# Windowed attention and a two-layer ReLU6 block: the matmuls in 64-row halves, two tiles at a time, and the sums copied out by VectorE alone

## The chip, the cores and the metric

The kernel runs on one core of a Trainium2 chip. The metric is the device time of the whole launch, in microseconds (us), as the median of several runs; a profiled execution of the same program shows what each engine did. TensorE (PE; its weight loads are shown as PEld), VectorE (DVE), ScalarE (ACT), GpSimd (POOL) and the queue of SyncE (SP) run side by side and wait for each other by semaphores only.

## What is computed

```python
def _attn_ref(x, weight_gen):            # x (4, 4096, 192), weight_gen (4, 4096, 8, 7)
    w = softmax(weight_gen, axis=-1)     # 7 taps for each token and head
    x_unf = windows of 7 tokens ending at each token, zero before the start
    return np.einsum('bshk,bskhg->bshg', w, x_unf).reshape(4, 4096, 192)

def _moe_ref(x, w_in, w_out):            # x (16384, 192), w_in (192, 2048), w_out (2048, 192)
    h = x @ w_in
    g = h * np.clip(h + 3.0, 0.0, 6.0) / 6.0
    return g @ w_out
```

The output is `_moe_ref` of the attention's result, in float32.

## The kernel before

**Tiling.** 16 pairs of groups (`PAIRS`) are worked through. A pair has 8 tokens on each of 128 partitions, and each of its two halves has 4 of them, 512 token columns (`N`). For a half, the attention's result is transposed to channels x tokens: block a (channels 0 to 127) in `xt_a`, block b (channels 128 to 191) in `xt_b`. The hidden size 2048 is cut into 16 tiles of 128 (`TILES`).

**Split numbers.** TensorE multiplies in float32r, a shortened float32. To keep precision every operand is stored as a high part and a low part (the remainder): `w_in`, `w_out`, `xt_a`, `xt_b`, `g_hi` and `g_lo`. ScalarE writes the high parts by a copy, VectorE the low parts by a subtraction.

**A tile.** `fill` (L464) makes h of a tile in one of four PSUM banks `work` by five matmuls of 512 columns: high x high, high x low and low x high of block a, then two for block b. In `xt_b` 64 rows hold high parts and 64 rows hold low parts, so that the first of these gives high x (high + low), the second low x (high + low). ScalarE takes relu(h + 3) out of the bank (L254), VectorE multiplies min(relu, 6) by h in the bank (`gate`, L350), ScalarE copies the high part to `g_hi` (L264) and VectorE the low part to `g_lo` (L361). `multiply` then adds the tile to four banks `sums`, one for each token: for each a matmul of 384 columns (L482, g_hi by w_out high and low side by side) and one of 192 (L484, g_lo by w_out high, onto the second 192 columns).

**A half.** 18 slots (`GROUP_SLOTS`): twelve tiles, the two transposes TA and TB for the next half (L444), four tiles. TensorE fills slot m + 3 (`AHEAD`), then multiplies slot m; a bank of `work` is free when its low part is done. When the last tile has been multiplied, ScalarE copies the first 192 columns of each `sums` bank times 1/6 into `out_stage` (L281), VectorE adds the second 192 times 1/6 (L381), and SP stores the result. In the next half, TensorE's first matmul into each `sums` bank waits for `out_staged`.

**Beside it.** GpSimd does the attention of the next pair (`attend`, L147 to L158), for which VectorE and ScalarE compute the softmax weights in steps laid at slots 4, 5, 7 and 8 (`SHIFT_AT`, `EXP_AT`, `SUM_AT`, `SCALE_AT`; L325 to L341). Each engine's order is the order in which its program is written; a loop `Fori` runs over the pairs.

Of the kernel before, what the change touches and what calls it, by code (L numbers as in the profile page):

```python
# [6 lines left out]
F32R = mybir.dt.float32r  # L7
# [3 lines left out]

# [13 lines left out]

# [7 lines left out]

# [35 lines left out]
def is_tile(m):  # L69
    return slot(m)[1] not in (TA, TB)  # L70

# [11 lines left out]
def transposes_done(q, m):  # L83

    return 2 + 4 * q + sum(not is_tile(i) for i in range(m + 1))
# [47 lines left out]

def attend(eng, t, prods, accs, half, t0, t1, step, steps, ready):

# [26 lines left out]

# [57 lines left out]

def gpsimd_program(nc, pool, t, s):
# [11 lines left out]
    with pool.Fori(1, PAIRS) as q:  # L233
        for half in range(2):
# [3 lines left out]
            pool.wait_ge(s.transposed, 4 * q - 2 + 2 * half)  # L238
            attend(nc.gpsimd, t, t.pool_prod, t.pool_acc, half, 0, GT, s.pool_step,
                   ATTN_STEPS * (2 * q + half), s.attn_ready)  # L240

def scalar_program(nc, act, dram, t, s):
# [4 lines left out]
    def relu(q, m, last=False):  # L249

        if skipped(m, last) or not is_tile(m):
            return
        act.wait_ge(s.filled, tiles_done(q, m))
# [3 lines left out]
    def hi_part(q, m, last=False):  # L257

        if skipped(m, last):
            return  # L260
        half, what = slot(m)
        if is_tile(m):
            act.wait_ge(s.gated, tiles_done(q, m))
            nc.scalar.copy(t.g_hi[:, m % BANKS, :], t.work[m % BANKS][:]).then_inc(s.g_hi_ready, 1)  # L264
        else:
            act.wait_ge(s.transposed, transposes_done(q, m))
            x_hi(1 - half, what, t.work[m % BANKS])
# [8 lines left out]
    def evacuate(q, half):  # L276

        act.wait_ge(s.stored[half], 16 * q + 16)
        for n in range(GT):
            act.wait_ge(s.sums_ready, GT * (2 * q + half) + n + 1)  # L280
# [3 lines left out]
    def step(q, m, last=False):  # L284
        relu(q, m + 1, last)
        if m == SLOTS - 1 + EVAC_LAG:
            evacuate(q, 0)
        if m == ROUND - 1 + EVAC_LAG:
            evacuate(q, 1)
        hi_part(q, m, last)  # L290
        if m == EXP_AT and not last:
            softmax_exp(q + 1)
# [13 lines left out]
    for i, what in enumerate((TA, TB)):  # L306
        act.wait_ge(s.transposed, i + 1)
        x_hi(0, what, t.work[BANKS - 2 + i])
    w_out_hi(1)
    relu(0, 0)  # L310
    for m in range(FIRST):
        step(0, m)
    with act.Fori(0, PAIRS - 1) as q:
        for m in range(FIRST, FIRST + ROUND):
            step(q, m)
    for m in range(FIRST, ROUND + EVAC_LAG):
        step(PAIRS - 1, m, last=True)

def vector_program(nc, dve, t, s):
# [22 lines left out]
    def gate(q, m, last=False):  # L344

        if skipped(m, last) or not is_tile(m):
            return
        bank = t.work[m % BANKS]
        dve.wait_ge(s.relu_ready, tiles_done(q, m))
        nc.vector.scalar_tensor_tensor(bank[:], t.relu[:, m % 2, :], 6.0, bank[:],  # L350
                                       ALU.min, ALU.mult).then_inc(s.gated, 1)

    def lo_part(q, m, last=False):

        if skipped(m, last):
            return
        half, what = slot(m)
        bank = t.work[m % BANKS]
        if is_tile(m):
            dve.wait_ge(s.g_hi_ready, tiles_done(q, m))  # L360
            nc.vector.tensor_tensor(t.g_lo[:, m % BANKS, :], bank[:], f32(t.g_hi[:, m % BANKS, :]),  # L361
                                    ALU.subtract).then_inc(s.g_lo_ready, 1)
        else:
            dve.wait_ge(s.xt_hi_ready, inputs_split(q, m))
            x_lo(1 - half, what, bank)
# [10 lines left out]
    def evacuate(q, half):  # L376

        for n in range(GT):
            stage = t.out_stage[:, half, n * D:(n + 1) * D]
            dve.wait_ge(s.main_staged, GT * (2 * q + half) + n + 1)  # L380
# [3 lines left out]
    def step(q, m, last=False):  # L384
        gate(q, m + 1, last)
        if m == SLOTS - 1 + EVAC_LAG:
            evacuate(q, 0)
        if m == ROUND - 1 + EVAC_LAG:
            evacuate(q, 1)
        lo_part(q, m, last)  # L390
        if last:
            return
        if m == SHIFT_AT:
            softmax_shift(q + 1)
        if m == SUM_AT:
            softmax_sum(q + 1)
        if m == SCALE_AT:
# [27 lines left out]
    gate(0, 0)  # L425
    w_out_lo(0)
    for m in range(FIRST):
        step(0, m)
    w_out_lo(1)
    with dve.Fori(0, PAIRS - 1) as q:  # L430
        for m in range(FIRST, FIRST + ROUND):
            step(q, m)
    for m in range(FIRST, ROUND + EVAC_LAG):
        step(PAIRS - 1, m, last=True)
# [3 lines left out]
def tensor_program(nc, pe, t, s):  # L438
    def transpose_set(half, what, bank):


        src = t.attn_a if what == TA else t.attn_b
# [195 lines left out]
```

## Time and profile before

| | |
|---|---|
| median of 3 runs | 1226.28 us (1226.02 to 1226.76) |
| span of the profiled execution | 1224.4 us |
| TensorE busy | 1194.6 us, 98% |
| VectorE busy | 803.7 us, 66% |
| ScalarE busy | 634.2 us, 52% |
| GpSimd busy | 690.8 us, 56% |
| moved by DMA | 42.08 MB, 34 GB/s |

The span runs from the first to the last instruction; the run's time holds 1.9 us more. Matmuls overlap in the records, and their ends are modelled: what a matmul costs is read from when the next one starts, not from its duration. The granted TensorE clock was full over all but the last slice of the span.

### The profile page before, as it was taken

To read this page: it belongs to the slowest core of one execution; us is meant where nothing else is said; L and a number is where in the kernel's file an instruction comes from. 1 tells how busy PE (TensorE), PEld (TensorE's weight loads), DVE (VectorE), ACT (ScalarE), POOL (GpSimd) and SP (SyncE) were. 2 spreads that over 40 slices of the span, in tenths; PEclk is the share of its full clock that TensorE was granted. 3 is DMA by queue.
4 is the path that set the end of the run, shared out by engine and by line. 5 is a ranking of instruction groups with operands and counts; after the bars stand their busy time and mean duration, and the time that the engine had idled before them with its cause. 6 is when DMAs were issued, how large, how long until landed. Compare 5 with 4: busy or idle time off the path is not lost.

```text
span 1224.4 us, 19650 instructions
## 1 busy us (share of the span) xinstructions
PE 1194.6 (98%) x6848; PEld 1083.3 (88%) x6848; DVE 803.7 (66%) x1362; ACT 634.2 (52%) x1269; POOL 690.8 (56%) x455
## 2 busy tenths in 40 slices
PE   1999999999999999999999999999999999999998
PEld 1899999999999999999999999999999999998997
DVE  7866657576665766656666575766657666566665
ACT  3455555455555555545555554555555555455554
POOL 7893854909358192762918549094581927729100
PEclk9999999999999999999999999999999999999999
DMA  6101010010101001010010100101010010100000
GB/s 179 46 22 58 20 45 13 20 58 20 58 0 65 14 20 58 0 65 13 20 58 20 45 13 20 58 20 58 0 56 22 20 58 0 65 13 13 13 14 13
DMA packets 12071, 42.08 MB, mean 34 GB/s; under 512 B 1183, under 2 KB 5279, under 8 KB 10139
## 3 DMA queue, kind: packets, MB, share of 16 engines
q1 hardware_dynamic: 12059, 41.93, 9.8%
q8 instruction: 7, 0.11, 0.0%
q14 instruction: 5, 0.04, 0.0%
HBM read 29.34 MB, written 12.58 MB: 34 GB/s over the span
## 4 chain that ended last, share of the span: by engine, by line
PE 96%; DVE 1%; POOL 1%; issue 0%; DMA 0%; ACT 0%; DVEq 0%; ACTq 0%
PE work L464 48%; PE sums L482 32%; PE sums L484 15%; PE work L444 2%; POOL pool_acc L154 0%; POOL pool_prod L152 0%; DVE w_in L404 0%; DMA w_raw<-weight_gen_dram 0%; DVE work L350 0%; DVE w_out L410 0%; DVE g_lo L361 0%; DVE out_stage L381 0%; POOL pool_acc L147 0%; POOL pool_prod L148 0%; DVE xt_b L373 0%
## 5 line engine op out<-in xcount | busy, mean ns | idle before, releaser
L350 DVE SCALAR_TENSOR_TENSOR work<-relu,work 128x512 f32<-128x512 f32 x512 | 355.2, 694 | 402.9 <-ACT relu L254 402.8
L482 PE MATMUL sums<-w_out,g_hi 128*128 128x384 f32 x2048 | 614.1, 356 | 0.7 <-DVE g_lo L361 0.7
L254 ACT ACTIVATE relu<-work 128x512 f32<-128x512 f32 x512 | 306.4, 598 | 554.0 <-PE work L464 549.3
L484 PE MATMUL sums<-w_out,g_lo 128*128 128x192 f32 x2048 | 513.0, 251 | 0.0
L464 PE MATMUL work<-xt_a,w_in 128*128 128x512 f32 x1536 | 449.3, 400 | 2.0 <-DVE xt_b L373 2.0
L482 PEld LDWEIGHTS sums<-w_out,g_hi 128*128 128x128 f32 x2048 | 384.3, 188 | 23.7 <-DVE g_lo L361 1.3
L484 PEld LDWEIGHTS sums<-w_out,g_lo 128*128 128x128 f32 x2048 | 389.8, 190 | 15.8
L361 DVE TENSOR_TENSOR g_lo<-work,g_hi 128x512 fp32r<-128x512 f32 x512 | 349.7, 683 | 2.1
L464 PE MATMUL work<-xt_b,w_in 128*128 128x512 f32 x1024 | 318.1, 392 | 0.0
L264 ACT CAST g_hi<-work 128x512 fp32r<-128x512 f32 x512 | 299.3, 585 | 11.4 <-DVE work L350 11.3
L147 POOL TENSOR_TENSOR pool_acc<-x_in,w_soft 128x768 f32<-128x768 f32 (+1 forms) x32 | 50.0, 1563 | 442.7 <-DVE w_soft L341 429.7
L154 POOL TENSOR_TENSOR pool_acc<-pool_acc,pool_prod 128x768 f32<-128x768 f32 (+1 forms) x160 | 295.6, 1847 | 0.0
L464 PEld LDWEIGHTS work<-xt_a,w_in 128*128 128x128 f32 x1536 | 255.6, 189 | 29.5 <-issue 2.3
L152 POOL TENSOR_TENSOR pool_prod<-x_in,w_soft 128x768 f32<-128x768 f32 (+1 forms) x160 | 249.2, 1557 | 0.0
L464 PEld LDWEIGHTS work<-xt_b,w_in 128*128 128x128 f32 x1024 | 192.8, 188 | 44.8
L148 POOL TENSOR_TENSOR pool_prod<-x_in,w_soft 128x768 f32<-128x768 f32 (+1 forms) x32 | 49.0, 1531 | 0.0
L444 PE MATMUL work<-ident,attn_a 128*128 128x128 f32 x128 | 19.7, 277 | 23.2 <-POOL attn_b L158 23.2
L158 POOL TENSOR_TENSOR attn_a<-pool_acc,pool_prod 128x512 f32<-128x512 f32 (+1 forms) x32 | 40.8, 1274 | 2.5
L381 DVE SCALAR_TENSOR_TENSOR out_stage<-sums,out_stage 128x192 f32<-128x192 f32 x128 | 36.6, 348 | 1.5 <-ACT out_stage L281 1.5
L444 PEld LDWEIGHTS work<-ident,attn_a 128*128 128x128 f32 x128 | 14.5, 143 | 23.2 <-issue 23.2
L281 ACT ACTIVATE out_stage<-sums 128x192 f32<-128x192 f32 x128 | 32.0, 346 | 1.8 <-PE sums L484 1.8
L373 DVE TENSOR_TENSOR xt_b<-work,xt_b 64x256 fp32r<-64x256 f32 x64 | 27.0, 422 | 2.0
(31 smaller groups left out, 203.7 us busy)
## 6 DMA issues: line engine op xcount, KB each, us to landing
x_in<-x_dram SPq DMA_DIRECT2D x15, 1344.0 KB, 6.0
out_dram<-out_stage SPq DMA_DIRECT2D x32, 384.0 KB, 2.8
w_raw<-weight_gen_dram SPq DMA_DIRECT2D x16, 224.0 KB, 3.0
w_out_raw<-moe_w_out_dram SPq DMA_DIRECT2D x1, 1152.0 KB, 13.5
x_in<-x_dram SPq DMA_DIRECT2D x1, 768.0 KB, 5.1
w_in_raw<-moe_w_in_dram SPq DMA_DIRECT2D x1, 768.0 KB, 8.9
w_in_raw<-moe_w_in_dram SPq DMA_DIRECT2D x2, 384.0 KB, 10.3
w_out_raw<-moe_w_out_dram SPq DMA_DIRECT2D x1, 384.0 KB, 6.6
```

What stands on the lines that cost most here:

```text
L147: eng.tensor_tensor(acc, x_tap(0), w_tap(0), ALU.mult).then_inc(step, 1)
L148: eng.tensor_tensor(prod[1], x_tap(1), w_tap(1), ALU.mult).then_inc(step, 1)
L152: eng.tensor_tensor(prod[k % 3], x_tap(k), w_tap(k), ALU.mult).then_inc(step, 1)
L154: eng.tensor_tensor(acc, acc, prod[(k - 1) % 3], ALU.add).then_inc(step, 1)
L254: nc.scalar.activation(t.relu[:, m % 2, :], t.work[m % BANKS][:], ACT.Relu, bias=3.0).then_inc(s.relu_ready, 1)
L264: nc.scalar.copy(t.g_hi[:, m % BANKS, :], t.work[m % BANKS][:]).then_inc(s.g_hi_ready, 1)
L350: nc.vector.scalar_tensor_tensor(bank[:], t.relu[:, m % 2, :], 6.0, bank[:], ALU.min, ALU.mult).then_inc(s.gated, 1)
L361: nc.vector.tensor_tensor(t.g_lo[:, m % BANKS, :], bank[:], f32(t.g_hi[:, m % BANKS, :]), ALU.subtract).then_inc(s.g_lo_ready, 1)
L444: ins = nc.tensor.transpose(bank[:, i * P:(i + 1) * P], src[:, half, i * P:(i + 1) * P], t.ident[:])
L464: ins = nc.tensor.matmul(bank[:], w, x, start=(i == 0), stop=(i == len(products) - 1))
L482: nc.tensor.matmul(t.sums[n][:, 0:2 * D], t.g_hi[:, m % BANKS, cols], t.w_out[:, j, :], start=(j == 0), stop=False)
L484: ins = nc.tensor.matmul(t.sums[n][:, D:2 * D], t.g_lo[:, m % BANKS, cols], t.w_out[:, j, 0:D], start=False, stop=(j == TILES - 1))
```

## The change

**TensorE.** Every matmul now takes 64 rows of its operands: rows 0 to 63 ("upper") or 64 to 127 ("lower"), `ROWS`. Two tiles make a duo. `fill_first(d)` issues the five products of tile 2d from the upper rows alternately with those of tile 2d + 1 from the lower rows; `fill_second(d)` then does the other half of each. The two halves so always write to different banks. The fifth product covers only those 256 columns whose high parts lie in the half's rows (`hi_b`), so that low x low is no longer computed. `multiply` handles (tile, part) items: for two `sums` banks at a time a matmul of each half with 384 columns, then one of each with 192; in the next part the halves trade banks. The transposes are halved in the same way. New waits stand on TensorE for its own earlier work: `filled_first` before `fill_second`, `turned` before each `multiply` but the one that starts a half, and `transposed_first`. A duo runs: wait for the bank, fill_first, multiply, fill_second, multiply. `g_hi` and `g_lo` have six buffers (`G_SLOTS`) for four.

**ScalarE and VectorE.** They work by duos: relu of both tiles, then both copies; both gates, then both low parts. The relu has scale 1/6 and bias 0.5, and the gate takes the minimum with 1. ScalarE no longer touches `sums`; VectorE takes each bank out by one `tensor_reduce` over both 192-column parts. The softmax steps are laid behind duos 2, 3, 4 and 5.

TensorE in the loop, a tile of before (its fill, the first two matmuls of its sums):

```order
L464 MATMUL work<-xt_a,w_in 128x512 x3
L464 MATMUL work<-xt_b,w_in 128x512 x2
L475 REGISTER_ALU
L482 MATMUL sums<-w_out,g_hi 128x384
L484 MATMUL sums<-w_out,g_lo 128x192
```

The same engine of after, the end of a `fill_first` and the `multiply` behind it (L501 and L537 upper and lower, L502 lower; x2 is one of each half):

```order
L501 MATMUL work<-xt_b,w_in 128x512
L502 MATMUL work<-xt_b,w_in 128x512
L501 MATMUL work<-xt_b,w_in 128x2x128
L502 MATMUL work<-xt_b,w_in 128x2x128
L524 ISA
L537 MATMUL sums<-w_out,g_hi 128x384 x2
L540 MATMUL sums<-w_out,g_lo 128x192 x2
```

One matmul has become two alternating ones, and the last product has 2 x 128 columns for 512. The program of TensorE has 1799 instructions for 909, that of the other engines is no longer than it was.

VectorE where the sums of the first half leave, before:

```order
L350 SCALAR_TENSOR_TENSOR work<-relu,work 128x512
L380 ISA
L381 SCALAR_TENSOR_TENSOR out_stage<-sums,out_stage 128x192
L380 REGISTER_ALU
L381 SCALAR_TENSOR_TENSOR out_stage<-sums,out_stage 128x192
```

and after:

```order
L363 ISA
L366 ISA
L367 TENSOR_REDUCE out_stage<-sums 128x192 x2
L366 REGISTER_ALU
L367 TENSOR_REDUCE out_stage<-sums 128x192 x2
L343 REGISTER_ALU
L344 SCALAR_TENSOR_TENSOR work<-relu,work 128x512
```

The four reductions stand ahead of both gates of the duo, where the adds stood between a gate and a low part.

```diff
+ROWS = [slice(0, DB), slice(DB, P)]
+def parts_after(d, second_fill):
+    h = d % HALF_DUOS
+    before, recent, new = 2 * d - 4, 2 * d - 3, 2 * d - 2
+    if second_fill:
+        return {1: [(recent, 1)], 2: [(before, 1), (recent, 1), (new, 0)],
+                TRANSPOSE_DUO: [(recent, 1)], TRANSPOSE_DUO + 1: [(before, 1), (recent, 0)],
+                TRANSPOSE_DUO + 2: [(new, 0)]}.get(h, [(recent, 1), (new, 0)])
+    return {2: [(before, 0), (recent, 0)], TRANSPOSE_DUO + 1: [(before, 0)],
+            TRANSPOSE_DUO + 2: [(recent - 2, 1)]}.get(h, [(before, 1), (recent, 0)])
 # ScalarE
-                             bias=3.0).then_inc(s.relu_ready, 1)
+                             bias=0.5, scale=1.0 / 6.0).then_inc(s.relu_ready, 1)
-            nc.scalar.mul(t.out_stage[:, half, n * D:(n + 1) * D], t.sums[n][:, 0:D],
-                          1.0 / 6.0).then_inc(s.main_staged, 1)
 # VectorE
-            nc.vector.scalar_tensor_tensor(stage, t.sums[n][:, D:2 * D], 1.0 / 6.0, stage,
-                                           ALU.mult, ALU.add).then_inc(s.out_staged, 1)
+            if n % 2 == 0:
+                dve.wait_ge(s.sums_ready, GT // 2 * (2 * q + half) + n // 2 + 1)
+            nc.vector.tensor_reduce(t.out_stage[:, half, n * D:(n + 1) * D],
+                                    t.sums[n][:, 0:2 * D].rearrange("p (o c) -> p c o", o=2),
+                                    AX.X, ALU.add).then_inc(s.out_staged, 1)
 # TensorE
+    def products(m, r):
+        rows = ROWS[r]
+        hi_b = bank.rearrange("p (i o c) -> p i o c", o=2, c=P)[:, :, r, :]
+        return [(bank[:], t.w_in[rows, 0, 0, cols], t.xt_a[rows, half, 0, :]),
+                (bank[:], t.w_in[rows, 0, 0, cols], t.xt_a[rows, half, 1, :]),
+                (bank[:], t.w_in[rows, 1, 0, cols], t.xt_a[rows, half, 0, :]),
+                (bank[:], t.w_in[rows, 0, 1, cols], t.xt_b[rows, half, :]),
+                (hi_b, t.w_in[rows, 1, 1, cols], block_b(t, half, r, r))]
+    def fill_first(q, d, last=False):
+        for i, (upper, lower) in enumerate(zip(products(2 * d, 0), products(2 * d + 1, 1))):
+            nc.tensor.matmul(*upper, start=(i == 0), stop=False)
+            ins = nc.tensor.matmul(*lower, start=(i == 0), stop=False)
+        ins.then_inc(s.filled_first, 1)
+    def fill_second(q, d, last=False):
+        pe.wait_ge(s.filled_first, duos_filled(q, d))
+        both = list(zip(products(2 * d + 1, 0), products(2 * d, 1)))
+        for i, (upper, lower) in enumerate(both):
+            ins_upper = nc.tensor.matmul(*upper, start=False, stop=(i == len(both) - 1))
+            ins_lower = nc.tensor.matmul(*lower, start=False, stop=(i == len(both) - 1))
+    def multiply(q, tiles, odd_first, turns, first=False, by_sets=False):
+        if turns is not None:
+            pe.wait_ge(s.turned, turns)
+        order = [(m, part, group) for m, part in tiles for group in range(2)]
+        if by_sets:
+            order = sorted(order, key=lambda o: o[2])
+        for i, (m, part, group) in enumerate(order):
+            sets = [(n, ROWS[(n + odd_first) % 2]) for n in (2 * group, 2 * group + 1)]
+            for n, rows in sets:
+                if j == 0 and part == 0 and not first:
+                    pe.wait_ge(s.out_staged, GT * 2 * q + GT * (m // SLOTS - 1) + n + 1)
+                nc.tensor.matmul(t.sums[n][:, 0:2 * D], t.g_hi[rows, m % G_SLOTS, n * P:(n + 1) * P],
+                                 t.w_out[rows, j, :], start=(j == 0 and part == 0), stop=False)
+            for n, rows in sets:
+                ins = nc.tensor.matmul(t.sums[n][:, D:2 * D], t.g_lo[rows, m % G_SLOTS, n * P:(n + 1) * P],
+                                       t.w_out[rows, j, 0:D], start=False, stop=last_part)
+    def duo(q, d, last=False):
+        bank_free(q, 2 * d - 3, last)
+        fill_first(q, d, last)
+        starts = d % HALF_DUOS == FIRST_DUO
+        multiply(q, parts_after(d, 0), 1, None if starts else turns_before(q, d, 0), by_sets=starts)
+        fill_second(q, d, last)
+        multiply(q, parts_after(d, 1), 0, turns_before(q, d, 1))
```

## Rows read from the trace of the kernel before

**Rows 1.** The page: span, then busy us (share of the span) and instructions of each engine.
```profile
span 1224.4 us, 19650 instructions
PE 1194.6 (98%) x6848; PEld 1083.3 (88%) x6848; DVE 803.7 (66%) x1362; ACT 634.2 (52%) x1269; POOL 690.8 (56%) x455
```
**Rows 2.** The page: the chain that ended last, shares of the span by engine and line.
```profile
PE 96%; DVE 1%; POOL 1%; issue 0%; DMA 0%; ACT 0%; DVEq 0%; ACTq 0%
PE work L464 48%; PE sums L482 32%; PE sums L484 15%; PE work L444 2%; POOL pool_acc L154 0%; POOL pool_prod L152 0%; DVE w_in L404 0%; DMA w_raw<-weight_gen_dram 0%; DVE work L350 0%; DVE w_out L410 0%; DVE g_lo L361 0%; DVE out_stage L381 0%; POOL pool_acc L147 0%; POOL pool_prod L148 0%; DVE xt_b L373 0%
```
**Rows 3.** The costliest groups: shapes, count | busy us, mean ns of one | idle before.
```profile
L350 DVE SCALAR_TENSOR_TENSOR work<-relu,work 128x512 f32<-128x512 f32 x512 | 355.2, 694 | 402.9 <-ACT relu L254 402.8
L381 DVE SCALAR_TENSOR_TENSOR out_stage<-sums,out_stage 128x192 f32<-128x192 f32 x128 | 36.6, 348 | 1.5 <-ACT out_stage L281 1.5
```
**Rows 4.** Timeline of one tile on TensorE: start us, us it took, engine, line, operands, count.
```profile
429.32 0.88 PE L464 MATMUL work<-xt_a,w_in 128*128 128x512 f32 x3
430.03 0.62 PE L464 MATMUL work<-xt_b,w_in 128*128 128x512 f32 x2
...
430.49 0.33 PE L482 MATMUL sums<-w_out,g_hi 128*128 128x384 f32 x1
...
430.66 0.25 PE L484 MATMUL sums<-w_out,g_lo 128*128 128x192 f32 x1
430.66 0.19 PEld L482 LDWEIGHTS sums<-w_out,g_hi 128*128 128x128 f32 x1
...
430.75 0.36 PE L482 MATMUL sums<-w_out,g_hi 128*128 128x384 f32 x1
430.77 0.19 PEld L484 LDWEIGHTS sums<-w_out,g_lo 128*128 128x128 f32 x1
430.94 0.25 PE L484 MATMUL sums<-w_out,g_lo 128*128 128x192 f32 x1
...
431.60 0.41 PE L464 MATMUL work<-xt_a,w_in 128*128 128x512 f32 x1
```
**Rows 5.** Timeline at the transposes of block a, and their costliest group's mean.
```profile
426.34 0.45 PEld L444 LDWEIGHTS work<-ident,attn_a 128*128 128x128 f32 x4
426.43 0.60 PE L444 MATMUL work<-ident,attn_a 128*128 128x128 f32 x4
...
L444 PE MATMUL work<-ident,attn_a 128*128 128x128 f32 x128 | 19.7, 277 | 23.2 <-POOL attn_b L158 23.2
L444 PEld LDWEIGHTS work<-ident,attn_a 128*128 128x128 f32 x128 | 14.5, 143 | 23.2 <-issue 23.2
```
**Rows 6.** Timeline of a middle tile on all engines: fill, relu, copy, gate, low part.
```profile
448.34 0.62 PE L464 MATMUL work<-xt_b,w_in 128*128 128x512 f32 x2
...
449.00 0.60 ACT L254 ACTIVATE relu<-work 128x512 f32<-128x512 f32 x1 [1.21 <-PE work L464]
...
449.63 0.70 DVE L350 SCALAR_TENSOR_TENSOR work<-relu,work 128x512 f32<-128x512 f32 x1 [1.00 <-ACT relu L254]
...
450.24 0.68 DVE L361 TENSOR_TENSOR g_lo<-work,g_hi 128x512 fp32r<-128x512 f32 x1
```
**Rows 7.** Who waited for whom: us in total, times, longest.
```profile
ACT relu L254 <- PE work L464: 549.3, 445, 2.8
POOL pool_acc L147 <- DVE w_soft L341: 429.7, 14, 31.2
```
**Rows 8.** Timeline where the sums of a half leave.
```profile
442.63 1.00 ACT L281 ACTIVATE out_stage<-sums 128x192 f32<-128x192 f32 x4
...
443.38 1.14 DVE L381 SCALAR_TENSOR_TENSOR out_stage<-sums,out_stage 128x192 f32<-128x192 f32 x4
```
**Rows 9.** Timeline of the end.
```profile
1220.10 1.16 DVE L381 SCALAR_TENSOR_TENSOR out_stage<-sums,out_stage 128x192 f32<-128x192 f32 x4 [1.46 <-ACT out_stage L281]
1220.25 0.25 PE L484 MATMUL sums<-w_out,g_lo 128*128 128x192 f32 x1
```
**Rows 10.** Timeline of the start: first relu, low part of w_out, a wait of TensorE.
```profile
29.20 0.60 ACT L254 ACTIVATE relu<-work 128x512 f32<-128x512 f32 x1 [1.49 <-PE work L464]
...
34.79 3.33 DVE L410 TENSOR_TENSOR w_out<-w_out_raw,w_out 128x2304 fp32r<-128x2304 f32 x1
...
39.36 0.44 PE L482 MATMUL sums<-w_out,g_hi 128*128 128x384 f32 x1 [0.73 <-DVE g_lo L361]
```

More of the change, by code:

```diff
@@ L305, in scalar_program @@
     w_in_hi(1)
-    for i, what in enumerate((TA, TB)):
-        act.wait_ge(s.transposed, i + 1)
-        x_hi(0, what, t.work[BANKS - 2 + i])
+    act.wait_ge(s.transposed_a, 1)
+    x_hi(0, TA, t.work[BANKS - 2])
+    act.wait_ge(s.transposed_b, 1)
+    x_hi(0, TB, t.work[BANKS - 1])
     w_out_hi(1)
-    relu(0, 0)
-    for m in range(FIRST):
-        step(0, m)
+    for d in range(FIRST_DUO):
+        duo(0, d)
     with act.Fori(0, PAIRS - 1) as q:
[L314 to L317, printed above, removed]
+        for d in range(FIRST_DUO, FIRST_DUO + DUOS):
+            duo(q, d)
+    for d in range(FIRST_DUO, FIRST_DUO + DUOS):
+        duo(PAIRS - 1, d, last=True)
 def vector_program(nc, dve, t, s):
@@ L424, in vector_program @@
     w_in_lo(1)
-    gate(0, 0)
     w_out_lo(0)
-    for m in range(FIRST):
-        step(0, m)
+    duo(0, 0)
     w_out_lo(1)
+    for d in range(1, FIRST_DUO):
+        duo(0, d)
     with dve.Fori(0, PAIRS - 1) as q:
[L431 to L434, printed above, removed]
+        for d in range(FIRST_DUO, FIRST_DUO + DUOS):
+            duo(q, d)
+    for d in range(FIRST_DUO, FIRST_DUO + DUOS):
+        duo(PAIRS - 1, d, last=True)
@@ L438, in tensor_program, with transposes @@
 def tensor_program(nc, pe, t, s):
-    def transpose_set(half, what, bank):
+    def transposes(half, what, bank, r):
         src = t.attn_a if what == TA else t.attn_b
-        for i in range(GT if what == TA else GT // 2):
-            ins = nc.tensor.transpose(bank[:, i * P:(i + 1) * P], src[:, half, i * P:(i + 1) * P], t.ident[:])
-        ins.then_inc(s.transposed, 1)
-    def fill(q, m, last=False):
+        rows = ROWS[r]
+        return [(bank[:, i * P + r * DB:i * P + (r + 1) * DB], src[rows, half, i * P:(i + 1) * P], t.ident[rows, rows])
+                for i in range(GT if what == TA else GT // 2)]
@@ L449, in fill, with bank_free @@
+    def bank_free(q, m, last=False):
         if skipped(m, last):
             return
[L451 to L462 removed]
@@ L463, in fill @@
[L463 to L487 removed]
+        if is_tile(m):
+            pe.wait_ge(s.g_lo_ready, tiles_done(q, m))
+        else:
+            pe.wait_ge(s.xt_lo_ready, inputs_split(q, m))
@@ L493, in tensor_program @@
+    transpose_second(0, t.work[BANKS - 2], t.work[BANKS - 1], 1)
     pe.wait_ge(s.w_in_lo, 1)
     pe.wait_ge(s.xt_lo_ready, 3)
-    for m in range(AHEAD + 1):
-        fill(0, m)
+    fill_first(0, 0)
+    fill_first(0, 1)
+    fill_second(0, 0)
+    fill_second(0, 1)
     pe.wait_ge(s.w_out_lo, 1)
-    multiply(0, 0, first=True)
+    multiply(0, [(0, 0)], 1, None, first=True)
     pe.wait_ge(s.w_in_lo, 2)
-    for m in range(1, EARLY):
-        fill(0, m + AHEAD)
-        multiply(0, m)
+    bank_free(0, 1)
@@ L503, in tensor_program @@
+    fill_first(0, FIRST_DUO)
+    multiply(0, [(1, 0)], 1, 1)
+    fill_second(0, FIRST_DUO)
+    multiply(0, parts_after(FIRST_DUO, 1), 0, 2)
     pe.wait_ge(s.w_out_lo, 2)
     with pe.Fori(0, PAIRS - 1) as q:
-        for m in range(EARLY, ROUND + EARLY):
-            fill(q, m + AHEAD)
-            multiply(q, m)
-    for m in range(EARLY, ROUND):
-        fill(PAIRS - 1, m + AHEAD, last=True)
-        multiply(PAIRS - 1, m, last=True)
+        for d in range(FIRST_DUO + 1, FIRST_DUO + 1 + DUOS):
+            duo(q, d)
@@ L514 @@
+    for d in range(FIRST_DUO + 1, DUOS + 2):
+        duo(PAIRS - 1, d, last=True)
 class Semaphores:
```

204 lines of the change are left out of this document (111 added, 93 removed).

## The prediction

> **What bounds the kernel now.** I read the page's busy line first, then the chain, the costliest groups, the timeline of one tile, the waits. TensorE is busy 98% of the span, VectorE 66%, ScalarE 52% [rows 1], and the chain that ended last is 96% TensorE: 48% in the fills (L464), 47% in the sums (L482, L484) [rows 2]. Busy time of pipelined matmuls is no proof, so the timeline is the better witness. In a middle tile the five fill matmuls take from 429.32 to 430.49 us, 1.17 us, and the eight of the sums from there to 431.60, 1.11 us, each starting on the heels of the last [rows 4]. A tile is 2.28 us; 512 tiles are 1167 us of 1224.4. The other engines wait for TensorE: ScalarE 549 us at the relu [rows 7]. So the end moves with TensorE's time per tile and with whatever makes TensorE wait.
>
> Two tile equations give what a matmul costs. A fill is 5 x 512 columns in 1.17 us, 0.234 each; a pair of the sums is 384 + 192 columns in 0.278. With a per column and b per matmul, 512a + b = 0.234 and 576a + 2b = 0.278, so a = 0.423 ns and b = 17 ns. There is a floor below which b isn't the word: the 128-column transposes start (0.60 - 0.28)/3 = 0.107 us apart and their weight loads (0.45 - 0.14)/3 = 0.103 [rows 5], where 128a would be 0.054. A load of weights takes about 0.107 us and the next one of the same rows waits for the matmul ahead of it; the load at 430.66 is followed by one at 430.77 [rows 4]. Even the pairs of the sums lean on it: 384a + 0.107 is 0.27 of their 0.278.
>
> **Part 1, the array in 64-row halves.** Each 128-row matmul becomes two of 64 rows, one in each half, written alternately and into different banks. If the halves run side by side, each half has the chain of loads and matmuls that the whole array had, and one step of a pair costs what one matmul costs now. The sums keep their columns: 4 x 0.278 = 1.11 us a tile. A fill keeps four steps of 512 columns, but the fifth, the low part of the weights with block b, now covers 256 columns, because each half takes only the high parts: low times low is dropped. Its price by a and b is 256a + 17 ns = 0.126 us; the bounds are 0.107 (the load) and 0.234 (the strided destination eats it all). I take 0.126, as the trace shows no reason for more: saved 0.108 us a tile, 512 x 0.108 = 55 us. Bounds of this term: 0 to 65 us.
>
> What the trace can't show is a 64-row matmul: [rows 4] has only whole-array ones. From below, b disappears under the other half's work; from above, halves don't overlap at all. Both are rivals below.
>
> Transposes: 6 a half before, 12 with 64 columns after. At 0.107 a step they cost the same if the halves overlap (6 steps); if not, 6 x 0.107 x 32 = 21 us more. I take nothing, as for the rest.
>
> New waits on TensorE. A bank must not be written by both halves at once, so each duo of tiles waits for filled_first and twice for turned. What each waits for lies one block back: between fill_first and fill_second stands a multiply of 0.56 to 1.1 us, between two multiplies a fill of 1.06, where a release takes 0.2 us (last fill matmul starts at 448.57, may stream 0.22, relu starts at 449.00 [rows 6]). Price nothing; at the shortest cover, 0.56 us, a release of 0.2 is still hidden. If that cover were gone it would be 0.2 x 3 x 256 duos, 150 us.
>
> **Part 2, duos.** Both tiles of a duo are filled together, at three quarters of the duo's time. The chain behind it: relu; gate 0.63 later; the next gate 0.60 after that; the copy of the second tile after its gate, 0.6; its low part 0.7 [rows 3, 6]. Written out from the fill's last column: 0.2 + 0.63 + 0.60 + 0.73 + 0.61 + 0.70 = 3.5 us for the odd tile, 2.9 for the even one. TensorE next wants the even low part after a multiply half, the next duo's fill, multiply and second fill: a whole duo (4.34 us) plus half a tile; and the odd one, for the bank, 1.1 + 4.34 = 5.4 us on. Cover 1.9 us, so nothing. What may be laid on top: the softmax steps, now one after each of duos 2, 4 and 5, are 1.3, 1.4 and 0.6 us of VectorE; x_lo 1.5. VectorE's own pace is 4 x 0.60 = 2.4 us a duo against 4.34 [rows 6], so each is caught up within a duo. GpSimd gets the softmax weights some three tiles (7 us) later; it waits 31 us a pair of halves for them now [rows 7], and its first half is needed some 20 tiles later against 22 us of work. Nothing.
>
> **Part 3, the sums leave by VectorE alone.** Off the list go four ScalarE copies and four VectorE adds of 192 elements a half; in come four reductions of 384. From 348 ns for 192 elements and 694 for 512 [rows 3] the slope is 1.08 ns, so 0.56 us each, starting 0.48 apart (0.27 now, (1.14 - 0.35)/3 [rows 8], plus 0.21). This is the one place where TensorE now waits. Let t be when the first two banks of sums end. Banks are free at t + 0.2 + 0.56 = 0.76, then 1.24, 1.72, 2.20. TensorE does the other two banks (0.28) and fill_first (1.06), asks for banks 0 and 1 at t + 1.34, and after two tiles' halves on them (0.56) for 2 and 3 at t + 1.90: the last comes at about 2.2, a wait of 0.3. Over 31 changes of half: 9.5 us. Before, the copy and add pipeline of 0.27 left no such wait [rows 8]. VectorE is held 2 us with the gates of the duo just filled queued behind; that duo's low parts come at 5.4 instead of 3.5, just inside the cover. The bounds: 0 if the reductions start 0.37 apart; 58 us if the stride of 192 elements in PSUM doubles them (rival D). The 1/6 moves from the copies to the relu's scale: same instruction, nothing.
>
> **Head and tail.** The first relu came after one fill [rows 10]; now fill_first of two duos and fill_second of one stand before it, three tiles of filling, and the low part of w_out (3.33 us) stands before duo 1's gates. TensorE was waiting 0.73 us there already [rows 10]. I count 2 us. At the end the last reductions come 0.5 us later than the adds [rows 9].
>
> **Sum, forecast A.** 1224.4 - 55 + 9.5 + 2 + 0.5 = 1181.4 us of span. The runs' median lies 1.9 above the span (1226.28), so 1183.
>
> **The rivals.**
> B, the fixed costs hide. While one half changes weights the other streams, so b goes: fill 2304 x 0.423 = 0.975 us; the pairs of the sums can't go below 384a + 0.107 = 0.27, so 1.08; a tile 2.055, 0.225 saved, 115 us. The wait at the change of half grows to 0.45 us (14). Time 1224.4 - 115 + 14 + 2.5 + 1.9 = 1128. For it: b isn't streaming. Against it: each half still has its own chain of load, matmul, load.
>
> C, slower: the loads queue. Twice as many loads of 128 columns, and if the loads of both halves go through one loader at 0.107 us, a pair of the sums has four of them, 0.43 us instead of 0.278; 1.71 a tile. A step of the fill has two, 0.21, under 0.234, so 4 x 0.234 + 0.21 = 1.15. A tile 2.86, 0.58 more, 297 us; transposes 21 more: about 1545. It decides as soon as loads of different halves are closer than 0.278/4 = 0.07 us apart at best. For it: no loads stand closer than 0.10 in [rows 5] and the loader is busy 6848 x 0.107 = 733 us now, 1470 then. Against it: all loads there fill the same 128 rows, each waits for the matmul before it, so they don't show one loader.
> The Trainium skill ("TensorE: Matmul & The Clock Gate", section LDWEIGHTS) has a load take columns / 1.2 ns whatever the number of rows, which the transposes' 0.107 agrees with; by that page alone halving the rows saves nothing on a load. The Trainium skill ("TensorEngine Tiling (Array Packing)", Key Properties) says that different tiles execute LdWeights and Matmul in parallel, which speaks for A; no run shown here has two tiles.
>
> D, the reductions are slow. A stride of 192 in PSUM at double price, 0.88 us apart: the last bank is free at 0.2 + 3 x 0.88 + 0.96 = 3.8, a wait of 1.9, 31 times 59 us instead of 9.5: 1232. It decides from about 0.4 us apart.
>
> E, feeding. Twice the matmuls through one queue. The closest two matmuls of these kinds start 0.08 to 0.09 apart [rows 4]; if that were the least for any two, the sums take 16 x 0.088 = 1.41 us instead of 1.11 and the fill 10 x 0.088 is still under 1.06: 0.3 - 0.108 more a tile, 98 us: 1325. Against it: those 0.09 are explained by columns and load.
> The Trainium skill ("TensorE: Matmul & The Clock Gate", Part 2, decode and dispatch) prices a decoded matmul at about 62 ns in the sequencer; by it 26 take 1.6 us a tile, and that would not bind at 2.17.
>
> F, the halves don't overlap: 26 matmuls one after another, 10 + 16 at today's spacings, 4.3 us a tile: 2250.
>
> **How the numbers follow.** A 0.44, B 0.18, D 0.09, E 0.10, C 0.15, F 0.04. The likeliest is A, 1183; it alone spans 1160 to 1205. The range is to leave out no more than 2 in 10: C and F are out, so from 1105 (B with a little more) to 1335 (E). A measurement of this kernel tells 0.2%, 2.5 us, from no change. Faster: A, B and some of D's milder forms, 0.66; within 0.2%: a corner of D, 0.03; slower 0.31.
>
> **What would show it.** Right: steps of the fill 0.23 apart in pairs that start within a few ns, the last 0.13; pairs of the sums 0.28; one wait of 0.3 us a half at L537 for VectorE. B: fill steps at 0.217. C: loads never under 0.1 apart, sums at 0.43. D: reductions over 0.9 us and waits of 2 us. E: all matmuls 0.088 apart. The forecast is wrong from the root if paired starts don't coincide.

## The result: 1.8% slower, and the profile after

| | before | changed |
|---|---|---|
| median | 1226.18 us (4 runs, 1226.02 to 1226.76) | 1248.03 us (4 runs, 1241.88 to 1255.40) |
| ratio, 95% interval | | 1.018, 1.014 to 1.022 |
| span of the profiled execution | 1224.4 us | 1239.9 us |

The forecast was 1183 us with 0.66 for faster. The time lies inside the range (1105 to 1335) and on the wrong side of no change. The changed kernel also scatters by 13 us where the old one scatters by 0.7.

The page after: its span and busy lines, the queue q8, which brings in instructions, and its chain. The first two lines answer to [rows 1], the last to [rows 2]; q8 had moved 7 packets for the kernel before:

```profile
span 1239.9 us, 33575 instructions
PE 1169.6 (94%) x13696; PEld 1094.8 (88%) x13696; DVE 841.8 (68%) x1362; ACT 633.3 (51%) x1141; POOL 690.7 (56%) x455
...
q8 instruction: 139, 2.28, 0.8%
...
PE 92%; DVE 4%; ACT 2%; issue 1%; POOL 1%; DMA 0%; DVEq 0%
```

TensorE is busy for 25 us less although the span is 15.5 us longer: its work became shorter, and time without work appeared. First the work. Two steps of a fill and the first matmuls of the sums, in the timeline (start us, us, engine, line, operands), which answers to [rows 4]:

```profile
430.80 0.39 PE L501 MATMUL work<-xt_a,w_in 64*128 64x512 f32 x1
...
430.81 0.39 PE L502 MATMUL work<-xt_a,w_in 64*128 64x512 f32 x1
...
431.03 0.39 PE L501 MATMUL work<-xt_a,w_in 64*128 64x512 f32 x1
...
431.49 0.27 PE L501 MATMUL work<-xt_b,w_in 64*128 64x256 f32 x1
...
431.50 0.27 PE L502 MATMUL work<-xt_b,w_in 64*128 64x256 f32 x1
...
431.60 0.34 PE L537 MATMUL sums<-w_out,g_hi 64*128 64x384 f32 x2
431.61 0.19 PEld L540 LDWEIGHTS sums<-w_out,g_lo 64*128 64x128 f32 x2
431.78 0.26 PE L540 MATMUL sums<-w_out,g_lo 64*128 64x192 f32 x2
...
431.87 0.36 PE L537 MATMUL sums<-w_out,g_hi 64*128 64x384 f32 x2
```

The two halves start 0.01 us apart, so they do run side by side. A step of the fill is 0.23 us, the last 0.11; a pair of the sums (384 and 192 columns) is 0.27 here and 0.28 in the mean of the block before it. The sums here start at 431.60 and those of the previous block at 429.43: a tile is 2.17 us, which is the forecast's number (2.28 - 0.108).

Now the time without work. This is the timeline of TensorE where its loop over the pairs turns, from the last matmul of one turn to the first of the next:

```profile
343.95 0.24 PE L540 MATMUL sums<-w_out,g_lo 64*128 64x192 f32 x1
346.68 0.49 PE L501 MATMUL work<-xt_a,w_in 64*128 64x512 f32 x1 [2.48 <-DVE g_lo L349]
346.68 0.50 PE L502 MATMUL work<-xt_a,w_in 64*128 64x512 f32 x1
```

There are 14 such stops, one for each jump back (15 turns, and the last one's branch isn't taken), of 2.3 to 3.3 us from the start of one matmul to the start of the next, 38 us in all. Nothing in [rows 4 to 10] foretold them. The waits name two causes for them (who waits <- for whom: us in all, count, longest):

```profile
PEld work L501 <- DVE g_lo L349: 33.1, 36, 2.9
PE work L501 <- DVE g_lo L349: 26.4, 11, 2.6
...
PEld work L501 <- issue: 11.7, 4, 3.3
PE work L501 <- issue: 8.5, 3, 3.0
```

11 stops are put down to VectorE's low parts, 3 to "issue". Stops that come at the same place in every turn should have one cause; which, was the first question.

### The profile page after: what moved, and what is told of

It reads as the page before. It is cut to its first block, busy times and chain, and to the rows that moved or that the text cites. A ratio compares the mean times of both kernels' runs of the same rounds, so it can differ in the third digit from the quotient of the medians.

```text
span 1239.9 us, 33575 instructions
## 1 busy us (share of the span) xinstructions
PE 1169.6 (94%) x13696; PEld 1094.8 (88%) x13696; DVE 841.8 (68%) x1362; ACT 633.3 (51%) x1141; POOL 690.7 (56%) x455
## 2 busy tenths in 40 slices
DMA packets 12202, 44.24 MB, mean 36 GB/s; under 512 B 1183, under 2 KB 5279, under 8 KB 10139
## 3 DMA queue, kind: packets, MB, share of 16 engines
q8 instruction: 139, 2.28, 0.8%
## 4 chain that ended last, share of the span: by engine, by line
PE 92%; DVE 4%; ACT 2%; issue 1%; POOL 1%; DMA 0%; DVEq 0%
PE sums L537 35%; PE work L501 19%; PE work L515 18%; PE sums L540 11%; PE work L516 5%; PE work L502 3%; DVE g_lo L349 2%; DVE work L344 1%; ACT g_hi L266 1%; ACT relu L261 1%; PE work L453 1%; PE work L466 1%; POOL pool_acc L166 0%; POOL pool_prod L164 0%; DVE w_in L402 0%
## 5 line engine op out<-in xcount | busy, mean ns | idle before, releaser
L537 PE MATMUL sums<-w_out,g_hi 64*128 64x384 f32 x4096 | 664.5, 356 | 4.0 <-DVE g_lo L349 3.3
L540 PE MATMUL sums<-w_out,g_lo 64*128 64x192 f32 x4096 | 577.2, 249 | 0.0
L344 DVE SCALAR_TENSOR_TENSOR work<-relu,work 128x512 f32<-128x512 f32 x512 | 331.0, 692 | 323.0 <-ACT relu L261 320.4
L261 ACT ACTIVATE relu<-work 128x512 f32<-128x512 f32 x512 | 278.3, 596 | 447.7 <-PE work L516 447.7
L537 PEld LDWEIGHTS sums<-w_out,g_hi 64*128 64x128 f32 x4096 | 474.9, 185 | 25.8 <-DVE out_stage L367 6.9
L540 PEld LDWEIGHTS sums<-w_out,g_lo 64*128 64x128 f32 x4096 | 476.7, 187 | 0.0
L501 PE MATMUL work<-xt_a,w_in 64*128 64x512 f32 x768 | 230.8, 407 | 37.3 <-DVE g_lo L349 26.4
L164 POOL TENSOR_TENSOR pool_prod<-x_in,w_soft 128x768 f32<-128x768 f32 (+1 forms) x160 | 248.3, 1552 | 0.0
L502 PE MATMUL work<-xt_a,w_in 64*128 64x512 f32 x768 | 231.3, 407 | 0.0
L516 PE MATMUL work<-xt_a,w_in 64*128 64x512 f32 x768 | 226.5, 401 | 0.0
L515 PE MATMUL work<-xt_a,w_in 64*128 64x512 f32 x768 | 226.1, 400 | 0.0
L501 PEld LDWEIGHTS work<-xt_a,w_in 64*128 64x128 f32 x768 | 123.9, 187 | 53.4 <-DVE g_lo L349 33.1
L502 PE MATMUL work<-xt_b,w_in 64*128 64x512 f32 (+1 forms) x512 | 130.1, 334 | 0.0
L501 PE MATMUL work<-xt_b,w_in 64*128 64x512 f32 (+1 forms) x512 | 130.0, 333 | 0.0
L515 PEld LDWEIGHTS work<-xt_a,w_in 64*128 64x128 f32 x768 | 123.7, 186 | 6.3
L516 PE MATMUL work<-xt_b,w_in 64*128 64x512 f32 (+1 forms) x512 | 129.2, 331 | 0.0
L515 PE MATMUL work<-xt_b,w_in 64*128 64x512 f32 (+1 forms) x512 | 129.1, 331 | 0.0
L502 PEld LDWEIGHTS work<-xt_a,w_in 64*128 64x128 f32 x768 | 123.9, 187 | 0.1
```

Source lines behind the costliest of these rows:

```text
L164: eng.tensor_tensor(prod[k % 3], x_tap(k), w_tap(k), ALU.mult).then_inc(step, 1)
L501: nc.tensor.matmul(*upper, start=(i == 0), stop=False)
L502: ins = nc.tensor.matmul(*lower, start=(i == 0), stop=False)
L515: ins_upper = nc.tensor.matmul(*upper, start=False, stop=(i == len(both) - 1))
L516: ins_lower = nc.tensor.matmul(*lower, start=False, stop=(i == len(both) - 1))
L537: nc.tensor.matmul(t.sums[n][:, 0:2 * D], t.g_hi[rows, m % G_SLOTS, n * P:(n + 1) * P], t.w_out[rows, j, :], start=(j == 0 and part == 0), ...
```

## Two theories

**Theory 1, the fetch.** TensorE's program doubled, from 909 to 1799 rows, and with it the body of its loop. The engine no longer holds all of it; when the loop jumps back, its first block has to be brought in again. q8's 139 packets of 16 KB are the sign.

**Theory 2, VectorE.** The four reductions stand before the gates of the duo ahead of the loop's end, so the low parts come late and TensorE waits for its bank.

Against theory 2 speaks the middle of each pair: the same reductions stand there too, and TensorE doesn't stop. The trace speaks against it too. These are the last low parts before the stop's end (346.68):

```profile
344.54 1.29 DVE L349 TENSOR_TENSOR g_lo<-work,g_hi 128x512 fp32r<-128x512 f32 x2
```

They are done at 345.83, 0.85 us before TensorE goes on. At the 14 stops this lead is 0.4 to 1.4 us, so it isn't the low part that ends them.

## Experiments on the stops

**The loop written out.** The edit, in TensorE's program only:

```diff
-    with pe.Fori(0, PAIRS - 1) as q:
+    for q in range(PAIRS - 1):
         for d in range(FIRST_DUO + 1, FIRST_DUO + 1 + DUOS):
             duo(q, d)
```

> The changed kernel with TensorE's loop over the pairs written out, so that its program never jumps back; nothing else differs. Theory 1 (fetch): the changed trace stops TensorE for 2.3 to 3.3 us once a pair, 15 times, right after the loop's last matmul, and the instruction queue q8 moved 139 packets where it moved 7; the body no longer stays in the instruction memory. Written out, the stops go: 15 x 2.6 = 39 us less, about 1205 us, and faster than the kernel before. Theory 2 (VectorE): the profile puts 26.4 us of these stops down to the low parts g_lo; then writing out changes nothing and the time stays at 1242 to 1255 us with a stop each pair.

Measured: 1200.3 us (4 runs, 1199.15 to 1203.59), ratio to before 0.980 (0.978 to 0.981). The page and its queue:

```profile
span 1197.3 us, 32405 instructions
PE 1162.8 (97%) x13696; PEld 1101.6 (92%) x13696; DVE 841.8 (70%) x1362; ACT 633.8 (53%) x1141; POOL 690.9 (58%) x455
...
q8 instruction: 107, 1.75, 0.6%
```

Theory 2 falls: VectorE does the same work in the same order (841.8 us), and the stops are gone, with 48 us of median. The 107 packets, in a trace without a stop, show that bringing in code costs nothing visible by itself: written out, all of it is fetched, but in a straight line. What costs is the jump.

**Control: the same edit on the kernel before.**

> Control: the kernel before with the same loop of TensorE written out. Its page had 7 packets on q8 and its pairs follow each other every 74.42 us without a stop, so both theories expect no change, 1226 us. If it gets faster, the kernel before paid at its loop's end too; if it gets slower, a written-out program costs something by itself.

Measured: 1226.19 us, ratio 1.000 (0.999 to 1.001). The old loop cost nothing at its end. Written out, it moves 53 packets on q8; the 7 of the looped kernel lie before 111 us and behind 1170 us, none of them between the jumps.

**The kernel before with a long body.** Three pairs in the body, 5 turns:

```diff
-    with pe.Fori(0, PAIRS - 1) as q:
-        for m in range(EARLY, ROUND + EARLY):
-            fill(q, m + AHEAD)
-            multiply(q, m)
+    with pe.Fori(0, (PAIRS - 1) // 3) as q3:
+        for i in range(3):
+            for m in range(EARLY, ROUND + EARLY):
+                fill(3 * q3 + i, m + AHEAD)
+                multiply(3 * q3 + i, m)
```

> The kernel before with three pairs in the body of TensorE's loop and 5 turns for 15: the same instructions in the same order, but a body of about 2800 instructions instead of 940. Theory 1: each of the 5 turns (4 or 5 jumps back) stops TensorE for 2 to 3 us, 10 to 13 us in all, about 1238 us, and q8 moves well over a hundred packets. Theory 2: no change, 1226 us.

Measured: 1230.08 us, ratio 1.003 (1.002 to 1.004): slower by 3.7 us, a third of what was expected. Four stops appear, one at each jump, in a kernel that had none (0.7, 0.8, 0.7 and 1.2 us from start to start), with 66 packets on q8. So the length of the body is enough, but a jump costs 0.9 us here and 3.4 in the changed kernel (47.7 / 14), with stops of 0.9 and 2.7 on the mean. Why, the branch's own row shows. For one source line the profile gives op, count, shortest/median/longest ns and the first and last start. The kernel before, then this one, then the changed kernel:

```profile
L505 PEldq COMPARE_BRANCH  x15: 76/208/247, 114.5 to 1156.2; - x15
```
```profile
L505 PEldq COMPARE_BRANCH  x5: 83/3296/3780, 263.6 to 1160.1; - x5
```
```profile
L575 PEldq COMPARE_BRANCH  x15: 83/3838/4365, 114.8 to 1169.0; - x15
```

The branch takes 0.2 us where its target is at hand, 3.3 to 4.4 us where it isn't, and 0.08 us on the last turn, when it isn't taken. Two more records tie the stop to the branch. At each of the 14 jumps of the changed kernel a packet of q8 starts 0.9 to 1.1 us behind the start of the branch. And the first matmul starts 0.16 to 0.17 us after the branch ends, at one of the 14 0.23 us. While the branch waits, TensorE works off what its queue holds. In this kernel the first branch starts at 263.6 us and TensorE runs dry after the matmul at 266.34:

```profile
266.34 0.25 PE L484 MATMUL sums<-w_out,g_lo 128*128 128x192 f32 x1
267.13 0.95 PE L464 MATMUL work<-xt_a,w_in 128*128 128x512 f32 x3 [0.53 <-issue]
```

That is 2.7 us of queued work; in the changed kernel the branch of the stop above starts at 342.68 and the last matmul at 343.95, 1.3 us. In both, 16 or 17 matmuls start between the start of the branch and the stop. So the halved matmuls hurt twice: the body grew beyond what is held, and the same number of queued instructions covers half as much of the fetch.

**The same in the fastest kernel.** It is the changed kernel with TensorE's loop written out and the old way out of the sums (1188 us, see below), with the loop put back, three pairs in a body:

> The fastest kernel so far (1188 us: written out, old way out of the sums) with TensorE's loop put back, three pairs in its body: 5 turns, 4 jumps back. If the cost is one fetch for each jump taken, it is 4 x 2.6 = 10 us, and up to 4 x 3.7 = 15 us where the stop also halves the clock for a while: 1198 to 1203 us, with four branches of 3 to 4 us and the fifth, not taken, short. If the cost went with the length of the body or with the number of blocks fetched, it would be near that of the body of one pair, 1243 us.

Measured: 1203.85 us, ratio 0.982 (0.980 to 0.984), 15.7 us above the same kernel written out. Its branch:

```profile
L585 PEldq COMPARE_BRANCH  x5: 83/3627/3862, 256.0 to 1128.5; - x5
```

Four jumps cost 3.9 us each, 14 cost 3.4 us each in the changed kernel (47.7 / 14), 3.9 each with the old way out of the sums (1243.2 - 1188.1 = 55 / 14). The cost goes with the jumps taken, not with the code fetched: 119 packets here, 107 written out. The expectation of 1198 to 1203 us was missed by 1 us.

Part of it is the clock. Stretches of the changed kernel's span, with the granted clock as the third column from the end, before, behind and after one stop:

```profile
180.00:191.20 11.20, 11.20 (x132) 10.19 (x128) 8.44 (x16) 5.67 (x11) 0.00 (x0) 1.00 0.38 146
194.95:198.30 3.35, 3.35 (x26) 3.15 (x25) 0.00 (x0) 0.00 (x0) 0.00 (x0) 0.53 0.00 0
200.00:210.00 10.00, 10.00 (x130) 9.37 (x127) 7.70 (x14) 6.06 (x11) 0.00 (x0) 1.00 0.01 2
```

Behind the stop of 191.1 to 193.7 us TensorE stood at 1.2 GHz for 3.4 us, half of 2.4, which costs it up to 1.7 us. Two of the 14 stops of this execution were followed by such a stretch (those of 2.6 us; the longest, 3.3 us, was not). The four runs' times go with their mean granted clock: 1241.9 us at 0.996, 1247.9 and 1248.2 at 0.990, 1255.4 at 0.981. This is where the scatter comes from, and it is why the 48 us of median are more than the 38 us of stops.

## Experiments on the rest of the change

**The old way out of the sums, in the loop.** ScalarE copies 192 columns, VectorE adds 192, the 1/6 stays in the gate:

```diff
+            nc.scalar.copy(t.out_stage[:, half, n * D:(n + 1) * D], t.sums[n][:, 0:D]).then_inc(s.main_staged, 1)
...
-            nc.vector.tensor_reduce(t.out_stage[:, half, n * D:(n + 1) * D],
-                                    t.sums[n][:, 0:2 * D].rearrange("p (o c) -> p c o", o=2),
-                                    AX.X, ALU.add).then_inc(s.out_staged, 1)
+            dve.wait_ge(s.main_staged, GT * (2 * q + half) + n + 1)
+            nc.vector.scalar_tensor_tensor(stage, t.sums[n][:, D:2 * D], 1.0, stage,
+                                           ALU.mult, ALU.add).then_inc(s.out_staged, 1)
```

> The changed kernel with the old way out of the sums: ScalarE copies the first 192 columns, VectorE adds the second 192 (the 1/6 stays in the gate). If the four reductions of VectorE are what makes TensorE wait at the change of half (0.25 us in the trace) and what puts its two row halves 0.09 us out of step for the following duos (0.066 us a duo), some 0.25 to 0.6 us a half come back: 8 to 19 us less than the changed kernel run beside it (about 1242 to 1248), while the stops at the loop's end stay. If the stops at the loop's end were made by the reductions ahead of the gates (theory 2), they shrink too: up to 39 us more.

Measured: 1243.17 us (1240.15 to 1248.46), ratio 1.014 (1.011 to 1.018). That is 5 us under the changed kernel, less than the 8 to 19 expected, and inside its scatter: by itself inconclusive. Its clock says why:

```profile
core 0: 1240.2 us, clock 0.984
```

All its four runs lie between 0.976 and 0.986. In the profiled execution nine of the 14 stops were followed by a stretch at half clock, one of them twice as long, 34 us in all. Here is the first and the long one:

```profile
118.80:122.10 3.30, 3.30 (x26) 3.06 (x24) 0.00 (x0) 0.00 (x0) 0.00 (x0) 0.50 0.00 0
...
569.40:576.10 6.70, 6.13 (x36) 5.42 (x38) 0.32 (x1) 0.00 (x0) 0.00 (x0) 0.50 0.01 2
```

The changed kernel had two such stretches, 6.8 us. The 27 us more at half clock cost up to 14 us, about what the old way out of the sums gives back below (12 us). Why more stops are followed by a slow stretch here stays open; their length doesn't decide it (2.3 to 3.3 us in both kernels). With the stops gone the part can be read:

**The old way out of the sums, written out.**

> The changed kernel, TensorE's program written out, with the old way out of the sums (ScalarE copies, VectorE adds). Theory: the reductions cost a wait of 0.25 us at each change of half and leave the two row halves 0.09 us out of step, 0.066 us a duo until the next transposes; both go, 0.3 to 0.6 us a half, 10 to 19 us: 1181 to 1190 us against about 1200. Rival: the steps out of step come from something else (the order by sets), and nothing changes.

Measured: 1188.13 us (1186.30 to 1189.53), ratio 0.969 (0.967 to 0.970), the fastest kernel of the study. The way out of the sums costs the written-out kernel 12 us. One change of half with the old way, on all engines:

```profile
362.57 0.26 PE L550 MATMUL sums<-w_out,g_lo 64*128 64x192 f32 x2
362.59 0.99 ACT L281 COPY out_stage<-sums 128x192 f32<-128x192 f32 x4 [2.04 <-PE sums L550]
...
362.94 1.15 DVE L378 SCALAR_TENSOR_TENSOR out_stage<-sums,out_stage 128x192 f32<-128x192 f32 x4 [1.67 <-ACT out_stage L281]
```

The four banks are free 1.5 us after the first copy starts, at 364.09 (362.94 + 1.15). Four reductions take 1.95 us, here in the changed kernel's timeline:

```profile
338.61 1.95 DVE L367 TENSOR_REDUCE out_stage<-sums 128x192 f32<-128x384 f32 x4 [1.31 <-PE sums L540]
```

In the written-out kernel that keeps the reductions TensorE waits for a bank at each change of half, by its waits:

```profile
PEld sums L537 <- DVE out_stage L367: 7.3, 31, 0.3
```

That is 7.3 / 31 = 0.24 us each, and it has a sequel. The bank that comes last belongs to one row half, so that only that half waits. Its timeline at one change of half (the reductions start at 327.07), in front of the wait, behind it, and eight microseconds later:

```profile
327.63 0.39 PE L501 MATMUL work<-xt_a,w_in 64*128 64x512 f32 x1
327.63 0.39 PE L502 MATMUL work<-xt_a,w_in 64*128 64x512 f32 x1
...
329.08 0.18 PEld L537 LDWEIGHTS sums<-w_out,g_hi 64*128 64x128 f32 x1 [0.23 <-DVE out_stage L367]
...
329.56 0.42 PE L516 MATMUL work<-xt_a,w_in 64*128 64x512 f32 x1
...
329.73 0.41 PE L515 MATMUL work<-xt_a,w_in 64*128 64x512 f32 x1
...
337.26 0.39 PE L502 MATMUL work<-xt_a,w_in 64*128 64x512 f32 x1
...
337.36 0.39 PE L501 MATMUL work<-xt_a,w_in 64*128 64x512 f32 x1
```

A pair of matmuls, one of each half, starts together before the wait, 0.17 us apart behind it, and still 0.10 apart eight microseconds on. From transposes to transposes a half takes 36.16 us with the reductions and 35.80 with the old way (mean of 30 each): 0.36 a half. 0.24 of it is the wait; the rest I put down to the ends of the blocks, where one half idles for the skew, which no run took apart.

**The reductions alone, in the kernel before.**

> The kernel before with part 3 alone: 1/6 in relu and gate, VectorE takes each bank of sums by one reduction, ScalarE no longer touches them. Theory: in the old order TensorE asks for a bank 1.2 us after its sums end, one bank each 0.28 us, and the four reductions, 0.48 us apart, keep ahead of that, so nothing changes: 1226 us. Rival: the reductions hold the low part queued behind them, 2 us for 1.1, and TensorE waits for it: up to 0.8 us a half, 1226 to 1250 us.

Measured: 1238.87 us, ratio 1.010 (1.009 to 1.012). My expectation missed; its rival holds in size, though not in what TensorE waited for. The waits name the banks, 62 times, not the low part:

```profile
PEld sums L471 <- DVE out_stage L369: 10.3, 62, 0.2
```
```profile
447.10 1.95 DVE L369 TENSOR_REDUCE out_stage<-sums 128x192 f32<-128x384 f32 x4
...
448.21 0.40 PE L471 MATMUL sums<-w_out,g_hi 128*128 128x384 f32 x1
...
448.63 0.45 PE L471 MATMUL sums<-w_out,g_hi 128*128 128x384 f32 x1
...
449.10 0.44 PE L471 MATMUL sums<-w_out,g_hi 128*128 128x384 f32 x1
```

TensorE would ask for a bank every 0.28 us and gets the last ones 0.42 and 0.47 us apart, the last at the reductions' own pace (0.47). I had let them start as soon as the sums end; a gate stood before them. So part 3 is a loss on its own, 12 us in the written-out kernel and 13 in the kernel before.

**Low x low computed again.** Written out; the fifth product over all 512 columns:

```diff
-                (hi_b, t.w_in[rows, 1, 1, cols], block_b(t, half, r, r))]
+                (bank[:], t.w_in[rows, 1, 1, cols], t.xt_b[rows, half, :])]
```

> The changed kernel, TensorE's program written out, with the fifth product of a fill over all 512 columns in both row halves, so that low times low is computed again: the size of the term 'low x low dropped' by itself. The forecast priced it at 0.108 us a tile, 55 us: about 1200 + 55 = 1255 us, which would be slower than the kernel before although its matmuls are all halved. If the halves hid their fixed costs (rival B) it would cost 256 columns x 0.423 ns = 0.108 as well, so the total tells nothing of B; the tile's length does: 2.28 us (A) or 2.16 (B).

Measured: 1248.18 us, ratio 1.018 (1.016 to 1.020), 48 us above its partner of 1200.3: the dropped product is worth 0.09 us a tile. Its tile (sums from 429.75, the next from 432.04) is 2.29 us, so forecast A's 2.28, not rival B's 2.16.

**The same with the old way out of the sums.**

> TensorE's program written out, the old way out of the sums, and low times low computed again over 512 columns: what is left of the change is the halving of the array and the order by duos alone, with the kernel before's columns. If halving gives and takes nothing in a tile (forecast A: each half repeats the old chain), this is the kernel before plus transposes and start: 1188 + 48 = 1236 us, about 10 above the kernel before. If halving hid fixed costs, it would be under 1226.

Measured: 1237.13 us, ratio 1.009 (1.008 to 1.011), as expected (1236). With the columns of the kernel before, halving the array is a loss of 11 us. One tile of it, on TensorE:

```profile
412.18 0.34 PE L546 MATMUL sums<-w_out,g_hi 64*128 64x384 f32 x2
...
413.29 0.41 PE L525 MATMUL work<-xt_a,w_in 64*128 64x512 f32 x1
413.30 0.41 PE L524 MATMUL work<-xt_a,w_in 64*128 64x512 f32 x1
...
414.47 0.33 PE L546 MATMUL sums<-w_out,g_hi 64*128 64x384 f32 x2
```

The sums take 1.11 us and the fill 1.18, as in [rows 4] (1.11 and 1.17). Halving hides nothing; all it buys is the dropped product.

## The prediction, step by step

| step | forecast | shown by | measured |
|---|---|---|---|
| a tile, halves side by side | 2.174 us | timeline after | 2.17 us |
| low x low dropped | -55 us | e1 - e5, e7 - e8 | -48, -49 us |
| reductions, waits at the change of half | +9.5 us | e1 - e7, e6 | +12, +13 us |
| new waits of TensorE on itself | 0 | waits after | 0.5 us, 3 times |
| transposes | 0 | e8 against before | 0.47 for 0.49 us a half |
| the rest of a half | 0 | e8 against before, a half 37.38 for 37.20 us | +5 us |
| head and end | +2.5 us | e8 against before | +5 us |
| loop's jump back | not in the sum | changed kernel - e1 | +48 us |

**Bounds and part 1 were right.** The chain of load, matmul, load is repeated in each half, as a and b from [rows 4] and [rows 5] had it, and the Trainium skill's statement that different tiles load and multiply in parallel ("TensorEngine Tiling (Array Packing)", Key Properties) agrees: loads of the two halves start 0.01 us apart (430.57 and 430.58 in this trace). The loads' length is unchanged by halving the rows: 185 to 187 ns for [64 x 128], 188 to 190 for [128 x 128]. Rivals B, C and F are excluded by the starts: B's fill step would be 0.217, C's pair of the sums 0.43, F's starts would not coincide. e8 shows it best, where a tile has the old columns and the old length. E is excluded too: matmuls of one half follow those of the other by 0.01. The 62 ns beside E are given by the Trainium skill ("TensorE: Matmul & The Clock Gate", Part 2) only for decoding in the sequencer's microcode; which decoding ran here, no trace shows.

**The term of the dropped product was too large**, 55 for 48 to 49. The fill itself gave what was priced: with the old way out of the sums it takes 1.069 us for 1.176 (means of some 450 fills of e7 and e8), 0.107 for 0.108. But the sums behind it take 1.122 for 1.114, so that 0.099 a tile is left, or (37.38 - 35.80) / 16.

**The reductions: right mechanism, low by 3 us.** The pace (0.47 us apart for 0.48) was right and the wait nearly (0.24 for 0.3); that the wait falls on one row half and leaves it behind wasn't seen. Rival D's pace of 0.88 is excluded.

**The transposes cost nothing, what stands behind them does.** In e8 the eight matmuls of the sums behind a half's second transposes take 0.75 us for 0.54 elsewhere, and the fill after them 1.25 for 1.17; the kernel before loses only 0.09 us there. Part 2 had the low parts ready 1.9 us early everywhere. This fill does wait for one, in most halves: 26 times, all of them here.

```profile
PEld work L510 <- DVE g_lo L361: 4.4, 26, 0.2
```

That is 0.17 us each. How much of the 5 us of the rest of a half it makes, no run took apart.

**What failed is a step that isn't there.** Part 1 counted the doubled matmuls by their time on the array, and rival E by the spacing of two. Neither asked where the instructions come from, and so the jump back of the loop, 48 us in the changed kernel, is in no term of the sum and in no rival. Without it (e1) the forecast's direction is right and its time 17 us low. The forecast's front said that the program goes from 909 to 1799 rows, and the page before has 7 packets on q8 for a program that turns 15 times, which means that the loop was held. The right question would have been what is late if it no longer is. The sum with what the runs showed: 1183 + 6 (product) + 3 (reductions) + 8 (rest of the halves, head and end: 10.7 for 2.5) = 1200, and e1 measured 1200.3; with 48 for the jumps, 1248. The terms are differences of these very runs, so that the sum closes proves nothing more. The price of a jump was in no row of the trace before: there a branch took 0.2 us.

**Head and end** were forecast at 2 and 0.5 us. The first transposes in the loop come at 54.3 us before and at 56.0 to 58.8 in the five kernels that I read it in (56.8 in the changed one, 56.1 in e8), 1.7 to 4.5 us later. From the last transposes to the end it is 54.0 us before and 57.4 in e8. Here TensorE's waits on itself show: in the changed kernel two of the three stand in the last 11 us, where one multiply follows another with no fill between.

**Not tried:** the softmax steps in their old places, and where between 930 and 1800 instructions the limit of the body lies.

## What to carry to other kernels

Count the instructions of a loop body before doubling them, and look at the instruction queue's packets and the branch's duration in the trace: here code that was no longer held cost 3 to 4 us at each jump back, less what the engine's queue covered, and small instructions cover little. A stop that follows a jump can be put down to a semaphore in the list of waits; writing the loop out tells the two apart with one edit. Splitting the array into row halves repeated its chain of loads in each half and hid none of it, so its worth here is the columns that it lets you drop.

## What the runs showed of the hardware

- A taken branch of TensorE's sequencer lasted 0.21 us when its target was held, 3.3 to 4.4 us when it was fetched, 0.08 us when not taken. A body of some 930 instructions was held, one of some 1790 not. These two numbers are estimates, worked out from the code, each load and each matmul counted: (32 blocks x 13 matmuls + 12 transposes) x 2 and some 70 waits and other instructions before, (32 x 26 + 24) x 2 and some 80 after.
- Straight-line code was fetched without a visible cost: 107 packets of 16 KB in 1197 us, one every 11 us, and no stop (e1).
- 16 to 18 matmuls start between the start of the branch and the stop. That is 2.7 us of full matmuls (e3) and 1.1 to 1.3 us of halved pairs.
- The two matmuls of a pair, one of each row half, start most often 3 to 10 ns apart in the changed kernel. Where one waited alone (e1), the halves were 0.17 us apart behind the wait and 0.10 eight microseconds later.
- Stops of 2.3 to 3.3 us were followed by 3.4 us at a granted clock of 1.2 GHz, once by 6.8: 2 of 14 in the changed kernel, 9 of 14 with the old way out of the sums.
